# A third early expert tile, of expert 0, in an attention, mixing and expert chain

## The reference, cut to what matters

```python
for b in range(B):                       # 4
    prev_e = -1
    for s in range(S):                   # 544 here
        fresh_e = int(np.argmax(logits[b, s]))
        if s == 0 or local_gate[b, s] < 0.5:
            e = fresh_e
        else:
            e = prev_e if prev_e >= 0 else fresh_e
        prev_e = e
        ...
        h = np.maximum(x[b, s] @ w1[e], 0.0)      # 512 -> 1024
        out[b, s] = p[e] * (h @ w2[e])            # 1024 -> 512
```

## Time and profile before

| what | value |
|---|---|
| time, median of 3 runs | 621.69 us (620.43 to 622.03) |
| the profiled execution's own time | 621.54 us |
| its span | 619.5 us |
| granted TensorE clock, mean | 0.999 |
| PE busy | 608.2 us (98%) |
| DVE busy | 410.9 us (66%) |
| ACT busy | 321.4 us (52%) |
| POOL busy | 178.9 us (29%) |

### The profile page before, as it was taken

How to read it: one execution, slowest core, us unless ns; L and a number is a source line. 1 busy time by engine, 2 the same in 40 slices (tenths; PEclk the granted TensorE clock), 3 DMA queues, 4 the chain that set the end, 5 groups by cost and what they waited for, 6 DMA issues and landing times.

```text
span 619.5 us, 14715 instructions
## 1 busy us (share of the span) xinstructions
PE 608.2 (98%) x4483; PEld 505.0 (82%) x4484; DVE 410.9 (66%) x1164; ACT 321.4 (52%) x698; POOL 178.9 (29%) x257
## 2 busy tenths in 40 slices
PE   8999999999999999999999999999999999999996
PEld 6878888888888888889979878788788888888885
DVE  4767779845888797786979958957736235463541
ACT  5767779777516614632544844637526125362531
POOL 4545545600000000000000331585732521544141
PEclk9999999999999999999999999999999999999999
DMA  8987886002210010000004661786933522764000
GB/s 308 377 278 245 266 284 219 18 2 86 63 74 0 1 51 18 0 34 35 0 23 166 239 235 51 287 306 215 339 124 118 201 65 84 251 208 144 17 17 15
DMA packets 32935, 84.66 MB, mean 137 GB/s; under 512 B 4602, under 2 KB 7418, under 8 KB 32896
## 3 DMA queue, kind: packets, MB, share of 16 engines
q1 hardware_dynamic: 26816, 70.03, 32.5%
q0 software_dynamic: 3200, 8.92, 4.3%
q10 hardware_dynamic: 2880, 5.24, 2.6%
HBM read 76.04 MB, written 9.70 MB: 138 GB/s over the span
## 4 chain that ended last, share of the span: by engine, by line
PE 93%; DVE 4%; issue 1%; ACT 0%; POOL 0%; DVEq 0%; POOLq 0%; ACTq 0%
PE banks L889 23%; PE banks L891 23%; PE banks L890 23%; PE banks L760 4%; PE banks L827 3%; PE banks L1079 3%; PE banks L836 2%; DVE we_lo L1531 2%; PE banks L790 2%; PE banks L774 2%; PE banks L804 1%; PE banks L800 1%; PE banks L998 1%; PE banks L851 1%; PE banks L792 1%
## 5 line engine op out<-in xcount | busy, mean ns | idle before, releaser
L1498 DVE CUSTOM_DVE_ANT_0 product<-x,xT 128x512 f32<-128x512 f32 x120 | 77.9, 688 | 1.4 <-DMA xT<-in_w 1.3
L1800 ACT ACTIVATE prob<-neg,negmax 128x160 f32<-128x160 f32 (+1 forms) x136 | 59.2, 436 | 29.9 <-DVE negmax L1209 20.2
L1778 DVE TENSOR_SCALAR hid<-banks 128x512 f32<-128x512 f32 x34 | 23.5, 691 | 72.7 <-PE banks L891 71.6
L1910 ACT ACTIVATE k_sum<-banks 128x512 f32<-128x512 f32 (+2 forms) x40 | 21.4, 534 | 88.2 <-PE banks L891 84.7
L889 PE MATMUL banks<-we_hi,hid_hi 128*128 (+1 forms) x160 | 66.6, 416 | 0.2 <-DVE hid_lo L1611 0.2
L889 PE MATMUL banks<-we_hi,xg_hi 128*128 (+1 forms) x160 | 64.7, 404 | 0.9 <-DVE we_lo L1531 0.9
L686 POOL MEMSET xg<- 128x1024 f32 x1 | 1.0, 953 | 218.6 <-ACT k_raw L1903 218.6
L891 PE MATMUL banks<-we_hi,hid_lo 128*128 (+1 forms) x160 | 62.6, 392 | 0.0
L891 PE MATMUL banks<-we_hi,xg_lo 128*128 (+1 forms) x160 | 62.6, 391 | 0.0
L890 PE MATMUL banks<-we_lo,hid_hi 128*128 (+1 forms) x160 | 62.5, 391 | 0.0
L890 PE MATMUL banks<-we_lo,xg_hi 128*128 (+1 forms) x160 | 62.4, 390 | 0.0
(11 more groups left out here) (295 smaller groups left out, 1471.3 us busy)
## 6 DMA issues: line engine op xcount, KB each, us to landing
xT<-in_w_e SPq DMA_DIRECT2D x36, 512.0 KB, 4.6
raw_end<-in_w_e SPq DMA_DIRECT2D x36, 512.0 KB, 5.0
qk<-in_qk_t SPq DMA_DIRECT2D x32, 448.0 KB, 6.3
vw<-in_v_t SPq DMA_DIRECT2D x32, 256.0 KB, 5.6
w_raw<-in_w_mix ACTq DMA_DIRECT2D x20, 256.0 KB, 3.9
x_rows<-x SPq DMA_DIRECT2D x17, 256.0 KB, 2.0
xT<-in_w SPq DMA_DIRECT2D x8, 256.0 KB, 3.4
vz<-in_v_z SPq DMA_DIRECT2D x8, 128.0 KB, 3.7
```

The costliest lines, as they stand in the source:

```text
L1498: dve.tensor_tensor_reduce(product[:, k % 2, :], x2[:, t, :], w9(e), 1.0, 0.0, ALU.mult, ALU.add, dot[:, t % 2, e:e + 1]).then_inc(dotted, 1)
L1778: dve.tensor_scalar(hid[:, D * h:D * (h + 1)], ps_h[:, h, :], 0.0, None, ALU.max).then_inc(hid_ready, 1)
L1800: act.activation(prob[:, t % 2, c], neg[:, c], ACT.Exp, scale=-1.0, bias=negmax[:, t % 2, k:k + 1], accum_out=rsum[:, t % 2, k:k + 1]).the ...
```

## The change

`EARLY` becomes 3, with a new `OF_MOST = 2` for the tiles of the first expert. The third early tile takes the tokens that expert 0 has among the first 12 token tiles, up to 128, less those that are already taken. `most_chosen` works out their places, and `early_onehots` is split in three (`early_places`, `early_slot_onehots`, `early_tile_onehots`). GpSimd collects this tile once the rows of tile 0 are turned. The rest reorders TensorE, VectorE and ScalarE around the last choice.

```diff
-EARLY = 2
+OF_MOST = 2
+EARLY = OF_MOST + 1
...
-FILL = {4: (5, 6, 6, 0), 3: (2, 7, 0)}
+FILL = {4: (5, 6, 6, 0), 3: (2, 5, 0)}
...
@@ gpsimd
-            for b in range(EARLY):
+            for b in range(2):
                 gather(b, b, NA * P)
+            pool.wait_ge(xg_turned, 1)
+            gather(2, 0, NA * P)
...
@@ tensor
-            turn_rows(2, 0, 1)
-            keep_clock(IDLE_TURNS // 4)
             other = slice(1, 2)
-            pe.wait_ge(we_lo_ready, VPARTS + PARTS // 2 + VPARTS)
             pe.wait_ge(xg_lo_ready, 4)
             pe.wait_ge(hid_ready, 5)
-            hidden(2, other, 0, range(DC)).then_inc(hid_summed, 1)
-            sum_gates()
+            pe.wait_ge(we_lo_ready, VPARTS + VPARTS + 3)
+            hidden(2, other, 0, range(3))
+            pe.wait_ge(we_lo_ready, VPARTS + VPARTS + PARTS // 2)
+            hidden(2, other, 0, range(3, DC)).then_inc(hid_summed, 1)
...
             turn_hidden(2, 1)
-            outputs(2, 1, other, range(1, FC)).then_inc(y_summed, 1)
+            sum_gates()
+            outputs(2, 1, other, range(1, 2))
+            pe.wait_ge(we_lo_ready, VPARTS + VPARTS + VPARTS)
+            outputs(2, 1, other, range(2, FC)).then_inc(y_summed, 1)
...
@@ vector, most_chosen
-                dve.tensor_copy(first_i[:], first_e[:]).then_inc(first_known, 1)
+                known = done(dve.tensor_copy(first_i[:], first_e[:]))
+                done(dve.tensor_scalar(to_third[:], is_first[:, 0:1], -float(OF_MOST * P), None, ALU.mult))
+                after(done(dve.tensor_copy(sums_of_zero[:], sums_by_expert()[:, :, 0, :])))
+                after(done(dve.tensor_tensor_scan(place_zero[:], first_c[:, 0, 0:NA], sums_of_zero[:, 1, :], 0.0,
+                                                  ALU.mult, ALU.add)))
+                after(done(dve.scalar_tensor_tensor(place_zero[:], place_zero[:], to_third[:], sums_of_zero[:, 1, :],
+                                                    ALU.add, ALU.subtract)))
+                after(done(dve.tensor_tensor(place_zero[:], place_zero[:], sums_of_zero[:, 0, :], ALU.add)))
+                after(known)
+                dve.scalar_tensor_tensor(in_third[:], place_zero[:], float(P), early.pick[:, 0, :], ALU.is_lt,
+                                         ALU.mult).then_inc(first_known, 1)
...
@@ early_places
+                dve.wait_ge(first_known, 1)
+                kept = done(dve.tensor_tensor(in_third[:], in_third[:], taken[:, 0:NA], ALU.is_gt))
                 after(slotted)
+                after(done(dve.tensor_tensor(moved[:], place_zero[:], slot_early[:], ALU.subtract)), kept)
+                after(done(dve.tensor_tensor(moved[:], moved[:], in_third[:], ALU.mult)))
+                done(dve.tensor_tensor(slot_early[:], slot_early[:], moved[:], ALU.add))
...
@@ the table
-            none_before = done(dve.memset(tile_e[:, 0, 0:1], -1.0))
+            none_before = done(dve.memset(tile_e[:, 0, 0:1], 0.0))
...
@@ the loop, vector
-            with dve.Fori(EARLY + 1, MT) as i:
+            with dve.Fori(EARLY, MT) as i:
```

More of the change, by code:

```diff
@@ L699, in _ @@
                 pool.wait_ge(x2_stored[t], 16 * sum(t < n for n in SIZES))
-            for b in range(EARLY):
-                pool.wait_ge(xg_turned, b + 1)
-                gather(EARLY + b, b, TOK)
+            pool.wait_ge(xg_turned, 2)
+            gather(3, 1, TOK)
             pool.wait_ge(xg_turned, 3)
             gather(4, 0, TOK)
-            for b in range(EARLY):
+            for b in range(2):
                 scatter(b, b)
@@ L1106, in _ @@
             turn_hidden(0, 0)
-            hidden(0, first, 1, range(2, 3))
-            turn_keeps(final)
-            hidden(0, first, 1, range(3, DC)).then_inc(hid_summed, 1)
+            hidden(0, first, 1, range(2, DC)).then_inc(hid_summed, 1)
             turn_rows(1, 1, 0)
@@ L1516, in rest_of_squares @@
                     else:
-                        to = min(at + (3 if tiles == GT else 1 if f < GT and last_group(g) else 2), left)
+                        to = min(at + (3 if tiles == GT else (0, 0, 0, 1, 2, 2, 2, 2)[f] if last_group(g) else 2), left)
                         dots(n0 - before, at, to)
@@ L1999, in _ @@
             round_hidden(2, 0)
+            relu_hidden(2, 1)
+            round_rows(3)
+            round_hidden(2, 1)
+            rounded_weights(2, slice(0, 1), range(3, 4))
             def weigh_y(b):
@@ L2005, in _ @@
             act.wait_ge(gates_ready, 1)
[L2006 to L2011 removed]
+            for b in range(2):
+                weigh_y(b)
+            rounded_weights(2, slice(0, 1), range(4, 6))
             def finish_y(i, b, before_it):
```

113 lines of the change are left out of this document (63 added, 50 removed).

## The result

The changed kernel took 638.65 us (median of 6 runs, 637.71 to 639.99), the kernel before 621.86 us (6 runs, 620.43 to 623.53). The ratio is 1.0272, with a 95% interval of 1.0251 to 1.0294: 16.8 us slower. The prediction had 634.2 us and a range up to 636.6. The direction and the largest term were right; the sum was 4.5 us short.

The account below looks back on a forecast made before the run. TensorE, busy 98% of the span, was taken to bound the kernel, with VectorE level at the loop's start. 621.54 + 12.36 (one more tile) + 0.3 (VectorE) = 634.2 us; range 631.6 to 636.6.

Parts of the forecast that it names:

- 21 tiles, +12.36: In the loop: the third early tile replaces no later one, so 21 tiles for 20, adding 12.36 us on TensorE.
- The gap between tiles 1 and 2: TensorE's 3.04 us there: `turn_rows` moves into tile 1, the other 2.6 us can go; tile 2 starts near 387.
- Early part, 0: Before tile 0: VectorE's 13 short instructions, about +2.1 us, and TensorE's 0.4 us wait are offset; together 0, bounds -0.3 and +1.5.
- Net +0.3 us: VectorE from the last logits to tile 3's relu: new waits less vanished ones give +0.3 us, bounds -2.4 and +2.4.
- removes no VectorE instruction: Last logits to tile 3's relu: the change only reorders VectorE's instructions, so TensorE arriving 3 us early would wait.
- The counts (0.3 to 1.1): In the last choice on VectorE: the counts' wait for TensorE was put at 1.3 us where 0.3 was.
- the gates (1.3 for 1.0): On VectorE ahead of the loop: `gates_summed` comes late, 1.0 us of idle.
- `hid_lo` (1.0 us less): On VectorE: part of the `hid_lo` waits goes, some 1.2 of 2.9 us.
- The waits for the carry: In the last choice on VectorE: the waits of `carry`, 0.6 us, go.
- it waits at `tables_ready` (then at about 401 to 402): At the loop's start: TensorE, 3 us early, waits for VectorE's table at about 401 to 402, or at `turn_hidden`.
- Rival D, the clock: Ahead of the loop's first `turn_hidden`: fillers gone, 2 to 4 us idle lowers TensorE's clock; +1.5 to +4, 636 to 638; chance 0.06.
- A: The forecast case: 21 tiles and VectorE sets the start of the loop; 633.0 to 635.6 us, chance 0.66.

Follow-up runs that it names:

- a6_dve_last: Changed kernel with the last two low parts of the first expert's weights moved from GpSimd to VectorE; 637.83 us, ratio 1.0261.
- a1: Changed kernel with the last tile left out of the table (20 tiles, 23 tokens of expert 7 not written); 626.38 us, ratio 1.0084.
- a2: Changed kernel with 24 filler transposes on TensorE after tile 2's outputs, in the idle time ahead of the loop; 636.27 us, ratio 1.0255.
- d5_three_gates: 20-tile kernel (third early tile the first expert's, old order on both engines) with the gates' sums moved earlier in tile 2; 619.40 us, ratio 0.9976.
- d2: Changed kernel with tiles 0 and 1 in the old order on TensorE and VectorE, expert 0's low parts behind the slots; 637.66 us, ratio 1.0279.
- d3: As d2, with the table built before the wait for the gates and the first expert's last low parts on VectorE, not GpSimd; 635.07 us, ratio 1.0209.
- a3: Changed kernel with the table's steps on VectorE moved ahead of the wait for the gates' sums; 636.25 us, ratio 1.0237.
- a6_all: Changed kernel with early table, r = 2 weights prepared in the loop, first expert's last low parts on VectorE; 635.12 us, ratio 1.0234.
- c2_order_all: As a6_all, with TensorE's steps of the last choice put back in the old order, on TensorE alone; 640.97 us, ratio 1.0320.

## Why the prediction was right in part

- **21 tiles, +12.36.** Right, and the reason that it is slower. 168 matmuls; 12.38 us a tile; 11.7 and 12.0 us in the two kernels with one tile less and two more.
- **The gap between tiles 1 and 2.** Right that it goes, too hopeful in size. The fillers and the wait for rows are gone, but tile 2 starts at 389.03 where I had 387, and its last output ends at 403.4 where I had about 401 (404.4 before). A wait of 1.2 us for `hid_lo` in tile 0, new with the change, took part of it; the rest is not assigned.
- **Early part, 0.** Right: T0 is 0.26 us later, the wait for `x` 0.4 as said.
- **VectorE, "Net +0.3 us".** This is the term that failed. From the last logits to the relu of tile 3 VectorE had 43.5 us with 40.0 busy; now it has 47.0 with 41.6 busy: 3.5 us more where I had 0.3. About half of it is busy time. I took "removes no VectorE instruction" to mean that their length stays. Two steps grew by 1.4 us (0.80 and 1.46 for the 0.56 and 0.29 that the trace of before had), since GpSimd's low parts, which start 361.59 - 359.29 = 2.30 us after T0 and not 1.34, now fell on them. a6_dve_last shows both short once GpSimd is quiet. The other 1.9 us are waits. The counts (0.3 to 1.1), the gates (1.3 for 1.0) and `hid_lo` (1.0 us less) went about as I had them. The waits for the carry did not go but grew from 0.6 to 0.9, and the relu now waits 0.5 us for TensorE, which the low clock had made slow. The sum itself had a slip as well: the terms that I listed, +1.0, +1.0, -0.6 and -1.2, less 0.1 to 0.3 for the earlier start, give about 0 and not +0.3.
- **Where on VectorE the time goes.** From T0 to the counts it is 13.77 us before and 17.51 after, from T0 to the table 40.95 and 44.63. The table is thus late by what the choice is late: between the two it takes 27.18 us (25.58 busy) before and 27.12 us (24.48 busy) after. The two low parts that moved from behind the counts into the choice (1.2 us each) bring nothing there: the wait for the gates is new, and an `xg_lo` and a `hid_lo` of 0.68 us each now stand ahead of the table. Before, they stood behind it, between the table and the six low parts (399.98 to 401.09 in the earlier trace rows); the description of the kernel before leaves them out.
- **"it waits at `tables_ready` (then at about 401 to 402)".** The place was right, the time 2 to 3 us early (403.92), and I did not add what lies between the table and the first matmul of the loop, 2.66 us, since the earlier trace rows have it hidden. a1, a2 and a6_dve_last, with the table last as well, have 2.71, 2.64 and 2.70.
- **Rival D, the clock.** I gave it 0.06 as a case apart. It came on top of A: an idle time of 3.1 us, then 0.62. With fillers in the gap it is 1.00 and 0.95 us are saved. D's condition (TensorE idle for 2 to 4 us, the fillers gone) was met by A's own forecast, so the price of the clock belonged into the sum: 635.2 us with the 0.95 that it measured, 635.7 with the least that I had for it (1.5). The runs are at 638.65, so this alone does not close the gap. The Trainium skill, "TensorE: Matmul & The Clock Gate", section "What's actually happening", has the clock halved after TensorE has idled, and the trace agrees.

With the loop's start cleared of all this (a2: the relu at 51.38 us from T0 against 48.87 before), VectorE's part is 2.5 us and the clock's 0.95; with T0 0.26, the loop 0.25 and the end 0.17 that makes the 4.1 us by which the spans differ beyond the tile. The runs' medians have 4.4; the other 0.3 is not assigned.

What stays open: the port was not tested apart (with GpSimd's parts at another moment, say); shown is only that the slowing goes with GpSimd's parts. Why the loop's tiles are 0.04 us longer in d5_three_gates was not followed up. That matched orders gain nothing with 21 tiles (d2 against the kernel after, d3 against a3 and a6_all) while they are needed with 20 is read from traces, not tested by a run of its own. Which waits lower the clock, and which do not, was not tested either.

## What to carry to other kernels

Count tiles before counting gaps: a tile split off early is worth its gap only if it takes one away at the end, and here it took 12 us to save at most 3.3. The order of a chain that crosses two engines is one thing written in two programs; put back in TensorE's alone it cost nearly 5 us more than changed in both, and put back in both it gained nothing by itself (1.0279 against 1.0272). Where a forecast makes an engine idle for some us at a place that was full, add the price of the clock and of the loop's entry to the same case, and look which transfers and which queued work the freed time runs into next.

## What was not expected of the hardware

- The granted clock fell after every idle stretch of 3.1 to 3.2 us ahead of the loop, in six kernels (the lowest window of 4 us had 0.50 to 0.78). It did not fall with waits of 0.6, 1.1 and 0.6 us some 4 us apart (a3_table), but it did after waits of 1.0 and 1.7 us that ended 2.5 us apart (c2_order_all, 0.57). After a wait of 2.1 us at the same line of the program it stayed at 1.00 in a6_all and was 0.57 in c2_order_all. The length of a single wait alone does not tell.
- Two short VectorE steps took 0.80 and 1.46 us beside GpSimd's `we_lo`, 0.17 and 0.30 without it. The kernel before had 0.56 and 0.29 at another overlap, and in d2_before_order a step that reads one tile took 1.24 us for 0.16.
- TensorE's first matmul of the loop came 2.63 to 2.71 us behind the table's last step in all seven kernels in which the table came last.
